# Chunked attention and two expert layers in fp32: the products with the values as 64x64 quarters in two banks

## What is computed

```python
for c in range(nc):                       # nc = 24 chunks of 32 queries
    q_c = q[:, :, c_start:c_end]
    k_full = np.concatenate([mem_k, k[:, :, l_start:r_end]], axis=2)
    v_full = np.concatenate([mem_v, v[:, :, l_start:r_end]], axis=2)
    scores = scale * np.matmul(q_c, k_full.transpose(0, 1, 3, 2))
    scores = scores - np.max(scores, axis=-1, keepdims=True)
    a = np.exp(scores)
    a = a / (np.sum(a, axis=-1, keepdims=True) + 1e-09)
    out[:, :, c_start:c_end] = np.matmul(a, v_full)
...
x = attention output as [3072 tokens, 512]
h = x @ w_in                              # 512 -> 2048
x = (h * sigmoid(h)) @ w_out              # 2048 -> 512
...                                       # then a soft mixture of 8 experts with 4 slots each
```

## Time and profile before

| | |
|---|---|
| three runs | 487.25, 489.22, 489.15 us; median 489.15 |
| profiled execution | 487.45 us, of which the span from the first to the last instruction 485.6 |
| mean granted TensorE clock | 0.981 of full speed |
| TensorE, matmuls | 458.2 us busy (94%) |
| TensorE, weight loads | 336.6 us (69%) |
| VectorE | 278.9 us (57%) |
| ScalarE | 137.7 us (28%) |
| GpSimd | 43.5 us (9%) |
| line 245, values | 28.5 us of matmuls in 768 records, 25.1 us of loads |

### The profile page before, as it was taken

The page is one execution under the profiler, slowest core; times in us unless marked ns, Lnnn a source line. Parts: engine busy times, 40 slices in busy tenths (PEclk is TensorE's granted clock), DMA queues, the critical chain, the costliest instruction groups (busy, mean ns, idle before and its releaser), DMA issues.

```text
span 485.6 us, 12250 instructions
## 1 busy us (share of the span) xinstructions
PE 458.2 (94%) x5456; PEld 336.6 (69%) x5456; DVE 278.9 (57%) x533; ACT 137.7 (28%) x253; POOL 43.5 (9%) x42
## 2 busy tenths in 40 slices
PE   6799999999999999999999999999999899999972
PEld 5688677677876787768777677776777768534541
DVE  5556557755586565766666765467464754732213
ACT  2465223233232323322233223222223211200102
POOL 2266100000000000000000000000000000000000
PEclk9799999999999999999999999999999999999986
DMA  8979222202230222202222022020005969999997
GB/s 338 385 267 392 101 99 100 93 26 79 99 99 13 88 99 99 99 3 97 101 99 67 33 99 100 0 88 1 2 1 214 395 267 430 423 361 426 424 347 267
DMA packets 19748, 81.59 MB, mean 168 GB/s; under 512 B 1648, under 2 KB 7920, under 8 KB 14064
## 3 DMA queue, kind: packets, MB, share of 16 engines
q1 hardware_dynamic: 19696, 80.81, 43.2%
HBM read 74.51 MB, written 6.29 MB: 166 GB/s over the span
## 4 chain that ended last, share of the span: by engine, by line
PE 83%; DMA 8%; DVE 5%; ACT 1%; issue 1%; DVEq 0%; SPq 0%; ACTq 0%
PE h_ps L263 53%; PE o_ps L245 6%; DMA unit<-w 5%; PE lpu_ps L277 5%; PE lpu_ps L297 3%; PE sx_ps L222 3%; DMA qk_sb<-qk 3%; PE pt_ps L231 2%; PE sx_ps L297 2%; PE h_ps L894 1%; PE pt_ps L836 1%; PE lpu_ps L285 1%; PE h_ps L629 1%; PE o_ps L874 1%; PE lpu_ps L307 1%
## 5 line engine op out<-in xcount | busy, mean ns | idle before, releaser
L263 PE MATMUL h_ps<-x_odd,wh 128*128 128x512 f32 x384 | 126.8, 399 | 0.0
L468 DVE SCALAR_TENSOR_TENSOR gT<-gT,h_ps 128x512 f32<-128x512 f32 (+1 forms) x108 | 66.5, 616 | 101.3 <-ACT gT L367 100.8
L367 ACT ACTIVATE gT<-h_ps 128x512 f32<-128x512 f32 (+1 forms) x108 | 58.5, 542 | 184.8 <-PE h_ps L263 184.7
L263 PEld LDWEIGHTS h_ps<-x_odd,wh 128*128 128x128 f32 x384 | 72.1, 188 | 20.6 <-issue 3.4
L263 PE MATMUL h_ps<-x_even,wh 128*128 128x512 f32 x256 | 85.0, 400 | 0.0
L263 PE MATMUL h_ps<-x_odd,wl 128*128 128x512 f32 x192 | 74.9, 390 | 0.0
L478 DVE STREAM_TRANSPOSE gB<-gT 128x512 f32<-128x512 f32 x80 | 56.7, 709 | 1.9
L263 PEld LDWEIGHTS h_ps<-x_even,wh 128*128 128x128 f32 x256 | 48.0, 188 | 13.4 <-issue 2.2
L263 PE MATMUL h_ps<-x_short,wh 128*128 128x256 f32 x256 | 51.9, 292 | 5.3 <-DVE gT L468 5.0
L725 POOL TENSOR_TENSOR sc<-sc,row_stats 128x512 f32<-128x512 f32 x24 | 25.0, 1044 | 314.9 <-DVE row_stats L452 314.9
L263 PE MATMUL h_ps<-x_even,wl 128*128 128x512 f32 x128 | 49.9, 390 | 0.0
(11 more groups left out here) (145 smaller groups left out, 499.0 us busy)
## 6 DMA issues: line engine op xcount, KB each, us to landing
unit<-w SPq DMA_DIRECT2D x32, 1024.0 KB, 11.7
qk_sb<-qk SPq DMA_DIRECT2D x24, 640.0 KB, 4.2
v_sb<-v SPq DMA_DIRECT2D x24, 512.0 KB, 5.1
w_stage<-w_in SPq DMA_DIRECT2D x4, 1024.0 KB, 9.4
wot<-w_outT SPq DMA_DIRECT2D x4, 1024.0 KB, 10.2
unit<-w_out SPq DMA_DIRECT2D x4, 1024.0 KB, 5.8
out<-unit SPq DMA_DIRECT2D x4, 1024.0 KB, 7.3
out<-unit SPq DMA_DIRECT2D x2, 512.0 KB, 5.3
```

What stands on the lines that cost most here:

```text
L263: last = nc.tensor.matmul(h_ps[k % 2][:, 0:TOKS[b]], w[:, n, kc, q * 128:(q + 1) * 128], x[:, lo, kc, 0:TOKS[b]], start=(kc == 0 and w is ...
L367: nc.scalar.activation(gt_of(b, k), h_ps[k % 2][:, 0:TOKS[b]], ACT.Tanh, scale=0.5).then_inc(tanh_done, 1)
L468: nc.vector.scalar_tensor_tensor(out=gt_of(b, k), in0=gt_of(b, k), scalar=1.0, in1=h_ps[k % 2][:, 0:TOKS[b]], op0=ALU.add, op1=ALU.mult).t ...
```

## The change

`pt` becomes [128, 16, 32], without the block-diagonal zeros. One matmul for each tile, head and chunk has 64x64 weights (the value rows of that chunk alone) and 32 moving columns: 32 a unit instead of 16. Chunk 0 uses the lower 64 rows of the array and writes `o_ps`, chunk 1 the upper 64 and writes `lu_ps`. So `lu_ps` has one more user, and waits and the order of `u_ps` change with it.

```diff
-        pt = at("pt", R + 1024, [128, 4 * PAIRS, QT])
+        pt = at("pt", R + 1024, [128, 4 * PAIRS, CHUNK])
...
-        u_ps = (lp_ps, s_ps, ex_ps, lu_ps)
+        u_ps = (lu_ps, lp_ps, s_ps, ex_ps)
...
             if dispatched:
-                pe.wait_ge(acc_done, 4 * dispatched - 1)
+                pe.wait_ge(acc_done, 4 * dispatched)
...
-        def pe_values(pe, u):
+        def pe_values(pe, u, dispatched=0):
...
             if u:
                 pe.wait_ge(x_done, u)
+            else:
+                pe.wait_ge(sc_done, 2)
+            if u == FIRST[2] - 1:
+                pe.wait_ge(w2t_cp, 1)
+            if dispatched:
+                pe.wait_ge(acc_done, 4 * dispatched - 3)
             for t in range(2):
                 for p in range(PAIRS):
-                    for h2 in range(2):
-                        a, r = place_of(p, h2)
-                        at, h = p * UT + t * QT, 2 * p + h2
-                        last = nc.tensor.matmul(o_ps[64 * h2:64 * h2 + 64, at:at + QT],
-                                                v_sb[:, u % V_RING, t, h * D:(h + 1) * D], pt[:, (2 * a + t) * 4 + r, :],
-                                                start=True, stop=True)
+                    for c in range(2):
+                        for h2 in range(2):
+                            a, r = place_of(p, h2)
+                            at, h = (2 * p + t) * CHUNK, 2 * p + h2
+                            last = nc.tensor.matmul((o_ps, lu_ps)[c][64 * h2:64 * h2 + 64, at:at + CHUNK],
+                                                    v_sb[64 * c:64 * c + 64, u % V_RING, t, h * D:(h + 1) * D],
+                                                    pt[64 * c:64 * c + 64, (2 * a + t) * 4 + r, :], start=True, stop=True)
             last.then_inc(o_mm, 1)
...
-                    pe.wait_ge(acc_done, 4 * b - 3)
+                    pe.wait_ge(acc_done, 4 * b - 2)
...
+            if values_at(b + 1, 0) is not None:
+                pe.wait_ge(x_done, values_at(b + 1, 0) + 1)
             nc.tensor.matmul(lu_ps[:, 0:TOKS[b]], fold[:], part[:, 0:TOKS[b]], start=True, stop=True).then_inc(fold_mm, 1)
...
-            pt_half(act, nc.scalar.copy, u, 0)
-            if u >= UNITS[0]:
-                pt_half(act, nc.scalar.copy, u, 1)
+            if u < UNITS[0]:
+                pt_half(act, nc.scalar.copy, u, 0)
+                return
+            act.wait_ge(p_tr, u + 1)
+            act.wait_ge(o_mm, u)
+            nc.scalar.copy(pt[:], pt_ps.rearrange("p (j q) -> p j q", q=CHUNK)).then_inc(pt_done, 2)
...
+        def x_chunk(u, c, i):
             b = max(b for b in range(NB) if FIRST[b] <= u)
+            return x_of(b)[:, i, :, :].rearrange("p k (t c q) -> p k t c q", c=2, q=CHUNK)[:, :, 2 * (u - FIRST[b]):2 * (u - FIRST[b]) + 2, c, :]
+
+        def o_chunk(c):
+            return (o_ps, lu_ps)[c][:, 0:2 * PAIRS * CHUNK].rearrange("p (k t q) -> p k t q", k=PAIRS, t=2)
 
         def act_x(act, u):
-            hi, lo = unit_x(u)
             act.wait_ge(o_mm, u + 1)
-            nc.scalar.copy(hi, heads(o_ps)).then_inc(xh_done, 1)
+            for c in range(2):
+                nc.scalar.copy(x_chunk(u, c, 0), o_chunk(c)).then_inc(xh_done, 1)
...
         def dve_x(dve, u):
-            hi, lo = unit_x(u)
-            dve.wait_ge(xh_done, u + 1)
-            nc.vector.tensor_tensor(lo, heads(o_ps), hi.bitcast(fp32), ALU.subtract).then_inc(x_done, 1)
+            for c in range(2):
+                dve.wait_ge(xh_done, 2 * u + c + 1)
+                last = nc.vector.tensor_tensor(x_chunk(u, c, 1), o_chunk(c), x_chunk(u, c, 0).bitcast(fp32), ALU.subtract)
+            last.then_inc(x_done, 1)
...
-            nc.vector.memset(pt[:], 0.0).then_inc(pt_zero, 1)
```

More of the change, by code:

```diff
@@ L162, in moe_program @@
         phi_in = sem("phi_in")
-        const_set, pt_zero, zeroed = sem("const_set"), sem("pt_zero"), sem("zeroed")
+        const_set, zeroed = sem("const_set"), sem("zeroed")
         wh_done, wl_first, wl_done = sem("wh_done"), sem("wl_first"), sem("wl_done")
@@ L330, in pe_block @@
                 if at_pause and values_at(b, n) is not None:
-                    pe_values(pe, values_at(b, n))
+                    pe_values(pe, values_at(b, n), b if k > dispatch_step(b) else 0)
                 if b and k == 1:
@@ L373, in pt_half @@
                 eng.wait_ge(o_mm, u)
-            else:
-                eng.wait_ge(pt_zero, 1)
             half = slice(64 * c, 64 * c + 64)
-            copy(pt[half, :, c * CHUNK:(c + 1) * CHUNK],
-                 pt_ps[half, :].rearrange("p (j q) -> p j q", q=CHUNK)).then_inc(pt_done, 1)
+            copy(pt[half, :, :], pt_ps[half, :].rearrange("p (j q) -> p j q", q=CHUNK)).then_inc(pt_done, 1)
         def act_pt(act, u):
-            pt_half(act, nc.scalar.copy, u, 0)
-            if u >= UNITS[0]:
-                pt_half(act, nc.scalar.copy, u, 1)
+            if u < UNITS[0]:
[4 more added lines that the diff above has]
+            nc.scalar.copy(pt[:], pt_ps.rearrange("p (j q) -> p j q", q=CHUNK)).then_inc(pt_done, 2)
         def act_exp(act, u):
```

3 lines of the change are left out of this document (removed).

## The result

Medians of 20 runs each: 489.02 us after (486.63 to 491.32), 485.92 us before (483.78 to 489.22). The means are 489.02 and 486.20 us. The ratio is 1.0058, 95% interval 1.0038 to 1.0078: the change costs 2.8 us (the medians alone lie 3.1 us apart), where I had forecast 0.25% less than before. That 489.02 lies only 1.0 us above my forecast of 488.0 is luck: the forecast started from a median of 489.15 us for before, of three runs, and over 20 runs that median is 485.92. What counts is the step from before to after, and its sign was wrong. The profiled execution took 489.12 us, its span 487.3.

What follows compares the result with a forecast made beforehand. TensorE bounds the full blocks; in block 0 its waits for VectorE's gate count too. Products -0.7, gate waits -0.3, first stage -0.2: -1.2 us, 486.2 profiled, median 488.0 (0.25% faster), range 484.0 to 491.5.

Steps and rivals of the forecast that it cites:

- The changed products: Values products on TensorE: a unit takes 1.12 us against 1.15, -0.7 us over 24 units.
- The round of about 60 ns: Values products: two records, one per 64-column half, take 60 ns; four quarters side by side would still take about 60.
- streaming: Rival for the values products: streaming, not loading, sets the round; -7.7 us over 24 units, median 481.0; 10%.
- my two candidates: What the values' round pays for: streaming 64 moving columns (52 ns) or loading 64 weight columns (54 to 57 ns).
- row halves in turn: Rival for the values products: row halves load one after the other, 2.06 us a unit, +21.8 us, median 510.4; 6%.
- a floor that costs a whole start: Rival for the values products: every short record costs 30 ns per start, about +22 us, median 511; 3%.
- The copies of the probabilities: Units 2 to 23: two ScalarE copies become one, 0.58 us back 22 times, costed at nothing on the path.
- The split of x: Copy and subtraction in halves: x 0.11 us earlier, -0.3 us at block 0's three gate waits, -0.2 in the first stage.
- The waits: New waits from sharing lu_ps and reordering u_ps: cost nothing while margins hold, at most 0.7 us once.
- the products as long as before and little else: The main forecast for the whole kernel, given 72%: values products last as long as before; median 488.0.
- the first rival: Streaming sets the values' round, so feeding at 10 ns a record limits: 0.83 us a unit, median 481.0; 10%.
- the first stage -0.2 us: Gain from the split of x before the first MLP step's wait of 0.32 us: twice 0.11 us.

Runs made afterwards that it cites:

- wide_first: The changed kernel, but each quarter product of units 0 and 1 streams its 32 columns twice; ratio to before 1.0081.
- after_clear: The changed kernel, with the three wot loads under way around 41 us issued behind step 8 of block 0; ratio to before 1.0044.
- short loads: Only a quarter of each of the four wot loads, in the changed kernel (ratio 1.0014) and in before (0.9973).
- quarters_first: Quarters in units 0 and 1 only, the old block-diagonal product in all other units; ratio to before 1.0051.
- wide_clear: The changed kernel with both the doubled streaming of wide_first and the later loads of after_clear; ratio to before 1.0009.
- busy_first: The changed kernel with 7 instead of 3 short matmuls between the values of unit 0 and of unit 1; ratio to before 1.0089.
- quarters_block0: Quarters in units 2 to 5 (block 0) only, the old product in all other units; ratio to before 1.0012.
- from2_clear: The old product in units 0 and 1, quarters in units 2 to 23, loads issued late as in after_clear; ratio to before 0.9997.
- shift_quarter: The changed kernel with 16 idle matmuls (64 instructions) added in an idle stretch at 12 us; ratio to before 1.0049.
- after_paced: The changed kernel with three wot loads issued one by one, behind steps 6, 8 and 10 of block 0; ratio to before 1.0098.
- quarters_early: Quarters and split x in units 0 to 5 only, the old product in units 6 to 23; ratio to before 1.0119.
- shift_whole: The changed kernel with 64 idle matmuls (256 instructions) added in an idle stretch at 12 us; ratio to before 1.0143.

## Why the prediction was wrong

**The changed products: right.** 1.14 us a unit against 1.12 forecast, loads of 135 ns, matmuls of 219 (196 was forecast; the record shrank by 3 ns, not by 26: the slope of 0.81 ns a column, taken between 64 and 512 columns, doesn't hold below 64, and this is the missing 0.02 us). The round of about 60 ns held with half the columns and with 64 again in wide_first, so streaming doesn't set it. What is left of my two candidates is loading the 64 weight columns; no run changed those, so a fixed cost of about 60 ns for each record on a tile is not excluded. Of the rivals, streaming, row halves in turn and a floor that costs a whole start are out.

**The copies of the probabilities: right.** ScalarE's 10.9 us less show nowhere on TensorE's path; no run changed the copies alone.

**The split of x: right.** 1.16 us; in after_clear the three waits for the gate are 2.7 us against 3.2, -0.17 each where I had said -0.11.

**The waits: right.** TensorE's waits have no row for the accumulation, for the copy behind `w2t_cp` or in front of the fold.

**The step that failed is the sum's tacit one, "the products as long as before and little else".** It priced 384 more matmuls at nothing once each was known to lie side by side with others. I weighed the feeding of instructions only as a pace, 10 ns a record in the first rival, and not as a supply in blocks; and I gave the first stage -0.2 us without asking what half as many columns do to its clock. Two costs stand in its place:

1. *Quarters in the first stage, at half clock.* That they cost is shown by swaps: put there alone they cost 0.51% (2.5 us), and taking them out of after_clear gave 0.47% back. As ratios this is most of the 0.58%. That the half clock is how rests on less: it is all that the trace of quarters_first has more of (10.2 us of it in all six kernels with plain quarters there and nothing added ahead, 0 to 6.8 in all with the old product), and wide_clear, where streaming twice ends it early, gave 0.35% back. wide_first and busy_first end it early too and were no faster than after; the gaps that they kept are the likely reason, see below.
2. *Gaps at the borders of instruction blocks.* Their mechanism is shown: they move with the count, appear with the old product, grow behind a load and go when the load is issued later. Their price is less certain. Clearing the one at 41 us took the ratio from 1.0058 to 1.0044, within the two intervals; short loads left the same 0.41%. Between wide_first and wide_clear it was 0.7%, clear of the intervals. quarters_block0, with one gap, lies at 1.0012. from2_clear has gaps of 1.0 and 1.8 us and no measurable loss, so a gap can cost less in the end than it is long; I have not shown what absorbs it.

**What the timed executions add.** The profile is of one execution, but the mean granted clock is on record for every timed one except those of before in the first comparison. One minus that clock, times the span, is the clock time withheld; a stretch at 1.2 GHz withholds half its length. In the 117 executions of before that ran beside the experiments, the time rises by 0.52 +- 0.06 us for each us withheld. With that slope, an estimate, the clock's share of each kernel's loss is (us, means, against the executions of before that ran beside it):

| kernel | longer by | withheld, more by | the clock's share | rest | gaps in the profile |
|---|---|---|---|---|---|
| quarters_first | 2.8 | 4.4 | 2.3 | 0.6 | none |
| after_clear | 1.7 | 3.3 | 1.7 | 0.0 | 0.8 |
| wide_clear | 0.3 | 0.4 | 0.2 | 0.1 | 1.1 |
| from2_clear | -0.4 | 0.3 | 0.2 | -0.5 | 1.0, 1.8 |
| shift_quarter | 2.4 | 3.5 | 1.8 | 0.6 | 1.0, 1.6 |
| wide_first | 2.9 | 1.6 | 0.8 | 2.0 | 0.5, 1.8 |
| busy_first | 3.8 | 2.8 | 1.5 | 2.3 | 0.4, 2.7 |
| after_paced | 5.4 | 5.7 | 3.0 | 2.4 | 3.7, 1.1 |
| quarters_early | 5.3 | 3.8 | 2.0 | 3.3 | 2.3 |
| shift_whole | 7.2 | 5.8 | 3.0 | 4.2 | 4.6, 2.0, 0.6 |

after had 8.7 us withheld, the five sets of before 5.4 to 6.3: 1.2 to 1.7 us of its 2.8 go with the clock, 1.1 to 1.6 are left for the gaps. By this estimate the two causes share after's loss about evenly, by the swaps the first stage has the larger part; the two readings are no closer than their noise allows. With the gap near 41 us cleared, the clock accounts for the whole of after_clear's loss. wide_first did win clock (busy_first hardly, over its timed executions), and both lost by what the clock doesn't explain: in this table a rest of 2 us or more stands only where the profile has a gap of 1.8 us or more that begins between 38 and 48 us. The slope is a correlation, it doesn't say in which stretch the clock was withheld, and the means carry 0.5 to 1.4 us of noise.

**What stays open.** quarters_early (1.0119) is dearer than quarters_first and quarters_block0 together (1.0063), and dearer than after, which has more quarters. The first need not add up: in quarters_block0 the first stage is 128 instructions shorter, the borders fall elsewhere, and its one gap, 1.4 us at 31 us, has no half clock behind it, while quarters_early has 2.3 us at 44. The second is not explained. Nor is the size of the rests: wide_first's profiled execution, with 2.3 us of gaps and no half clock ahead of 400 us, was 3 us faster than the median of its kernel, and whether the timed ones had longer gaps, one trace a kernel can't tell. In all other kernels with a gap of 1.6 us or more between 38 and 48 us, 3.4 us at half clock follow it (after has a granted clock of 0.84 from 41 to 52 us); wide_first has none.

## What to carry to other kernels

Count instructions, not only engine time: an fp32 matmul is four, and a stretch that issues 256 within 3 us can leave TensorE without instructions: 0.6 to 1.4 us here with DMA queues near idle, up to 4.6 with full ones. It needs longer work (a step of large matmuls) in the same block, and idle queues when the block begins. A load issued just ahead of such a stretch delays the instructions behind it. Splitting a product to skip its zeros gained nothing here (1.14 us a unit against 1.15), where the pace didn't follow the moving columns, and in a stretch where TensorE has idle time it came with a longer half clock.

## What I had not expected of the hardware

- TensorE's instructions come in packets of 16 KB, 256 each; where it had to stop, it went on 2.2 to 2.8 us after a packet's start, and the packet started 0.3 to 0.9 us after the block ahead of it was entered with idle queues, up to 4.8 with full ones.
- Quarters with 32 moving columns kept the granted clock at 1.2 GHz for 10.2 us in the first stage; with 64 columns, the instructions being the same, it was 0 and 3.4 us (one profile each).
- Halving the moving columns of a 64-column tile changed a matmul's record by 3 ns (222 to 219) and a unit's values by 0.01 us.
- In 117 executions of one kernel the time rose by 0.52 us for each us of clock withheld, that is by about a quarter of the time spent at 1.2 GHz.
